# Scores of two attention heads as one block-diagonal product instead of two tile products

## The reference, cut to what matters

```python
B, H, S, D = 2, 8, 768, 64;  block, window = (32, 16)
k_sum = k.reshape(B, H, nb, block, D).max(axis=3)
v_sum = v.reshape(B, H, nb, block, D).mean(axis=3)
scores_l = np.where(np.abs(i - j) < window, scale * q @ k.T, -1e9)
scores_s = scale * q @ k_sum.T + np.log(block)
a = softmax(concatenate([scores_l, scores_s], axis=-1))
x = (a @ concatenate([v, v_sum])).transpose(0, 2, 1, 3).reshape(B * S, H * D)   # 1536 x 512
h = np.maximum(x @ w_in, 0.0);  x = h * h @ w_out                               # 512 -> 2048 -> 512
h = x @ w_in2;  out = P(h) / (Q(h) + 1e-6) @ w_out2                             # cubic over quadratic
```

## Time and profile before

| | us |
|---|---|
| median of three runs | 622.54 |
| lowest, highest | 621.97, 623.78 |
| the profiled execution's own time | 623.78 |
| its span, first to last instruction | 622.1 |
| TensorE busy in the span | 594.0 (95%) |
| VectorE, ScalarE, GpSimd busy | 443.7, 262.2, 144.5 |
| bytes moved by DMA | 35.54 MB, mean 57 GB/s |
| query loads | 8, 384.0 KB each, median 5.4 us from issue to landing |

### The profile page before, as it was taken

The page is one execution under the profiler, slowest core; times in us unless marked ns, Lnnn a source line. Parts: engine busy times, 40 slices in busy tenths (PEclk is TensorE's granted clock), DMA queues, the critical chain, the costliest instruction groups (busy, mean ns, idle before and its releaser), DMA issues.

```text
span 622.1 us, 9784 instructions
## 1 busy us (share of the span) xinstructions
PE 594.0 (95%) x3264; PEld 486.2 (78%) x3264; DVE 443.7 (71%) x862; ACT 262.2 (42%) x553; POOL 144.5 (23%) x144
## 2 busy tenths in 40 slices
PE   5878989999999999999999989999999999999995
PEld 4766768888888888888888867778888888888884
DVE  5656679667343333356666599999999999999996
ACT  4757731111131111130111755556756666765663
POOL 5435450000030000030000465622222222222220
PEclk9989999999999999999999999999999999999999
DMA  8999856000000000022222300000100000100001
GB/s 239 232 196 239 182 194 249 0 1 0 1 0 0 0 0 0 0 68 99 82 92 100 101 1 0 1 0 1 68 0 0 0 0 0 68 0 1 0 1 67
DMA packets 26973, 35.54 MB, mean 57 GB/s; under 512 B 1856, under 2 KB 19264, under 8 KB 26944
## 3 DMA queue, kind: packets, MB, share of 16 engines
q1 hardware_dynamic: 24544, 33.96, 19.4%
q10 hardware_dynamic: 2400, 1.18, 0.9%
HBM read 30.80 MB, written 3.15 MB: 55 GB/s over the span
## 4 chain that ended last, share of the span: by engine, by line
PE 47%; DVE 35%; issue 11%; POOL 3%; DMA 1%; ACT 1%; DVEq 1%; POOLq 0%
PE bank L479 22%; PE bank L536 21%; DVE ratio L941 9%; DVE numer L923 6%; DVE ratio L935 5%; DVE numer L921 5%; DVE ratio L930 5%; DVE hhi L948 4%; POOL kwin L318 2%; PE bank L434 2%; POOL prob L340 1%; DMA vwin<-vsum 1%; PE bank L444 1%; PE bank L452 1%; PE bank L465 1%
## 5 line engine op out<-in xcount | busy, mean ns | idle before, releaser
L479 PE MATMUL bank<-xhi,whi 128*128 (+1 forms) x384 | 149.7, 390 | 1.2 <-DVE wlo L829 1.2
L479 PE MATMUL bank<-xlo,whi 128*128 (+1 forms) x384 | 149.4, 389 | 0.0
L479 PE MATMUL bank<-xhi,wlo 128*128 (+1 forms) x384 | 149.4, 389 | 0.0
L632 ACT ACTIVATE hsq<-bank 128x512 f32<-128x512 f32 x48 | 28.7, 598 | 218.6 <-PE bank L479 218.6
L394 POOL TENSOR_TENSOR denom<-denom,habs 128x512 f32<-128x512 f32 (+1 forms) x49 | 62.3, 1272 | 250.9 <-ACT denom L703 250.9
L479 PEld LDWEIGHTS bank<-xhi,whi 128*128 128x128 f32 x384 | 72.1, 188 | 16.3 <-DVE wlo L829 1.4
L479 PEld LDWEIGHTS bank<-xlo,whi 128*128 128x128 f32 x384 | 72.1, 188 | 15.0
L479 PEld LDWEIGHTS bank<-xhi,wlo 128*128 128x128 f32 x384 | 72.1, 188 | 15.0
L551 PE MATMUL bank<-whi,hhi 128*128 128x512 f32 x192 | 75.9, 395 | 7.6 <-DVE hlo L952 7.6
L536 PE MATMUL bank<-hhi,whi 128*128 128x512 f32 x192 | 74.8, 390 | 0.1
L551 PE MATMUL bank<-wlo,hhi 128*128 128x512 f32 x192 | 74.9, 390 | 0.0
(11 more groups left out here) (67 smaller groups left out, 889.2 us busy)
## 6 DMA issues: line engine op xcount, KB each, us to landing
wraw<-w SPq DMA_DIRECT2D x32, 512.0 KB, 3.6
kraw<-kT SPq DMA_DIRECT2D x8, 384.0 KB, 7.9
q<-qT SPq DMA_DIRECT2D x8, 384.0 KB, 5.4
vnat<-v SPq DMA_DIRECT2D x8, 384.0 KB, 7.0
vwin<-v SPq DMA_DIRECT2D x8, 384.0 KB, 5.7
out<-osb SPq DMA_DIRECT2D x12, 256.0 KB, 2.1
vwin<-v SPq DMA_DIRECT2D x16, 88.0 KB, 5.9
vwin<-vsum ACTq DMA_DIRECT2D x8, 144.0 KB
```

What stands on the lines that cost most here:

```text
L479: last = mm(hps[j % 2][:, :], W[a][:, j, kt * P:(kt + 1) * P], X[b][:, kt, bass.ds(CH * c, CH)], start=k == 0, stop=k == 3 * KT - 1)
```

## The change

The scores of both heads of a window become one product. The stationary operand is a 128x128 matrix with head 0's 64 queries in the upper left block, head 1's in the lower right and zeros elsewhere; the moving operand is the whole of `kwin` for that window. The output rows are the same as before.

The query tile becomes `qblk`, of 128 x 128 x 12 numbers, with the window as the last index, so that the 12 windows of one query column lie side by side; the host lays the queries out in the same way. A load is two DMAs, one per diagonal block, into 64 partitions each, and TensorE waits for 32 instead of 16. The zero blocks are cleared once: for the first batch element on VectorE, ahead of the clearing of `vwin` (`cleared` then counts to 3), for the second on GpSimd, after the first windows. TensorE's first three rounds are now a loop in the program instead of three copies.

```diff
-        q.append(area(f"q{s}", [P, S]))
+        qblk.append(area(f"qblk{s}", [P, P, NW]))
...
+    def clear_queries(engine, s, h):
+        engine.memset(qblk[s][QW * h:QW * h + QW, QW * (1 - h):QW * (1 - h) + QW, :], 0.0).then_inc(cleared, 1)
...
         def load_q(it, s):
-            sp.dma_start(q[s][:, :], pick(qT, it, s)).then_inc(q_in[s], 16)
+            for h in range(2):
+                sp.dma_start(qblk[s][QW * h:QW * h + QW, QW * h:QW * h + QW, :],
+                             pick(qT, it, s)[QW * h:QW * h + QW]).then_inc(q_in[s], 16)
...
-        sp.wait_ge(cleared, 1)
+        sp.wait_ge(cleared, 3)
         load_vwin(0, 0, False)
...
         pool.wait_ge(windows_ready, 1)
+        for h in range(2):
+            clear_queries(g, 1, h)
+            pool.wait_ge(cleared, 4 + h)
         windows(0, 1, first=True)
...
             if gi == 0:
-                pe.wait_ge(q_in[s], 16 * (it + 1))
+                pe.wait_ge(q_in[s], 32 * (it + 1))
...
-                for h in range(2):
-                    rows = slice(D * h, D * h + D)
-                    last = mm(sps[par][QW * h:QW * h + QW, u * COLS:(u + 1) * COLS], q[s][rows, QW * w:QW * w + QW],
-                              kwin[s][rows, w, :], start=True, stop=True)
+                last = mm(sps[par][:, u * COLS:(u + 1) * COLS], qblk[s][:, :, w], kwin[s][:, w, :],
+                          start=True, stop=True)
...
         scores(0, 0, 2)
-        for it in range(PAIRS - 1):
+        pe.wait_ge(cleared, 5)
+        with pe.Fori(0, PAIRS - 1) as it:
             attention(it, False)
...
             d.memset(kraw[s][:, BAND + S:], 0.0)
+        for h in range(2):
+            clear_queries(d, 0, h)
...
+    def by_query(t):
+        return np.ascontiguousarray(features_first(t).reshape(PAIRS, B, P, NW, QW).swapaxes(3, 4))
...
-    arrays = {"qT": features_first(q), "kT": features_first(k), "v": tokens_first(v),
+    arrays = {"qT": by_query(q), "kT": features_first(k), "v": tokens_first(v),
```

More of the change, by code:

```diff
@@ L112, in build @@
     half = FT // 2 * SLOT * 4
-    q, kraw, kwin, vwin, vnat = [], [], [], [], []
+    qblk, kraw, kwin, vwin, vnat = [], [], [], [], []
     for s in range(B):
         area = Area((W_HI, W_LO)[s] + half)
-        q.append(area(f"q{s}", [P, S]))
+        qblk.append(area(f"qblk{s}", [P, P, NW]))
         kraw.append(area(f"kraw{s}", [P, S + 2 * BAND]))
@@ L323, in windows @@
             if first:
-                pool.wait_ge(cleared, 1)
+                pool.wait_ge(cleared, 3)
             else:
@@ L519, in _ @@
         pe.wait_ge(consts, 4)
-        pe.wait_ge(cleared, 1)
+        pe.wait_ge(cleared, 3)
         scores(0, 0, 0)
```

## The result

| | before | changed |
|---|---|---|
| median, us | 623.16 | 642.05 |
| lowest to highest, us | 621.97 to 631.94 | 640.87 to 645.67 |
| span of the profiled execution, us | 622.1 | 640.1 |
| first feed-forward matmul starts, us | 83.08 | 99.69 |

A forecast was written before the change was run, and what follows sets the result against it. The change was to act only on the attention, the first 86 us, bound by DMA stalls and a second loop. Matmuls -1.2 and query loads +2.0, all else zero, made +0.8: 623.3 us, range 620.5 to 628.5.

The forecast's parts named there:

- the strided load: Score weight loads, columns 48 bytes apart: taken as hidden behind matmul records, zero cost, at most +0.83 us a group.
- the rival: Score weight loads: strided load shows, 0.4 us a group, 6.6 us in all, 629.1 us; chance 0.13.
- The matmuls: Score groups on TensorE: eight full-size records in the old time, 0.12 us gained a group by tile shape, -1.2 us.
- the first part of the prediction: What bounds the kernel: the change acts on the attention, first 86 us, its gain or loss passed on one for one.
- The query loads: Attention's query DMAs, two to 64 partitions for one to 128: 0.4 us each, five count, +2.0 us (0 to +4.2).
- The two later stalls: Attention outputs waiting for the summary broadcast: ends expected at 38.2 and 58.2 us for 37.23 and 56.74.
- Rival (a): Query DMAs: narrow loads pay in full, +5.0 on six loads, less 1.2 makes +3.8, 626.3 us; chance 0.2.
- The clearing and the loop: VectorE and GpSimd clearing zero blocks, TensorE's rounds as loop: both 0; uncovered 1.4 us, and 0.3 if branches show.
- Rival (c): Attention: matmuls count, loads do not, and the low clock after the second stall goes: -3.0, 619.5 us; chance 0.12.
- Rival (d): Scores on TensorE: the gap before scores stays and the loads cost their 2.0: 624.5 us; chance 0.1.

The follow-up runs named there:

- e1: Changed kernel, score matmuls reading 128 adjacent columns instead of columns 48 bytes apart (scores wrong): 625.13 us, ratio 1.0038 to the kernel before.
- e9: Changed kernel with one query DMA to all 128 partitions and adjacent stationary columns (scores wrong): 622.29 us, ratio 1.0007 to the kernel before.
- e3: Kernel before with each query load split into two DMAs, to partitions 0 to 63 and 64 to 127: 625.90 us, ratio 1.0065.
- e10: Changed kernel with one query DMA to all 128 partitions, column distance 12 kept (scores wrong): 640.66 us in one execution.
- e4: Changed kernel with TensorE's first three rounds unrolled again: 641.87 us, ratio 1.0315 to the kernel before.
- e6: Changed kernel with queries in blocks of two windows, stationary columns 8 bytes apart, true scores: 627.69 us, ratio 1.0060 to the kernel before.
- e7: Changed kernel with queries in blocks of four windows, stationary columns 16 bytes apart, true scores: 637.99 us, ratio 1.0230 to the kernel before.

## Why the prediction was wrong

**The step that failed** is in the part on the strided load: "A load may last as long as a record, 0.10 us, before it shows", and "A load twice as slow is still hidden". The condition was right. The size was not: the load takes 0.263 us from start to start, five times the 0.05 that the prediction had worked out for adjacent columns (e1 shows only that these take 0.111 or less), so 0.15 us shows on each of eight records. In all that is +1.24 us from scores to outputs (2.22 against 0.98 in e1_adjacent), where I took zero.

**The bounds failed too.** I took +0.83 a group as the upper end, from a score group at the low clock, and halved it for the rival. A slow clock is another mechanism, and its price bounds nothing about a load's reads. No row of before held a strided load; the honest upper end was open, and the range should have leant that way. The rival's arithmetic was sound (three groups with a summary, TensorE alone): with the measured 3.32 a group, 3 x 3.32 + 1.42 = 11.4 us against 8.28, +3.1 eight times, makes 25 us, and I had put +0.8.

**From 27 to 16.6 us.** The first two score groups take 4.62 us where they took 3.46, the other 22 cost 1.16 each: 26.7 us. Given back are TensorE's waits of before, 9.3 us before 115 (5.8 for vwin<-vsum of the earlier trace rows, and by the same view of groups 0.4 for VectorE, 2.4 for POOL, 0.7 for ScalarE), of which 1.2 remain, and the 1.6 us of low clock in the earlier trace rows. 26.7 - 8.1 - 1.6 = 17.0; measured 16.6. A slower TensorE hid the DMA that had limited the attention.

**The matmuls** were right in kind: eight records in the old time, the idle time of 0.17 gone, 0.49 for 0.58 from transposes to scores. The gain was 0.08 us a group and not 0.12: only the way into scores, 0.09, came back, and eight records take 0.98 us to the outputs where sixteen took 0.97. What reaches the median cannot be told from nothing (e9). And the attention's gain is not "passed on one for one", as the first part of the prediction has it: in e9 half of it went to the low clock behind it.

**The query loads** were mis-sized, within their range: +2.0 forecast, +4.0 in kernel before (e3, 2.2 to 5.9), and 2 to 3 beside adjacent full-size matmuls (e1 against e9, not clear of noise). In the changed kernel itself they cost about nothing, since nothing waits for them there (e10). The two later stalls that I expected to end at 38.2 and 58.2 us do not exist in it; e3 has them at 37.72 and 59.46. Rival (a) priced the loads at +5.0 and, less the matmuls, the whole at +3.8; measured are +4.0 for the loads alone and +2.4 (0.6 to 4.2) for the whole without the strided loads (e1). Both lie between its price and the forecast's, and the runs cannot choose.

**The clearing and the loop** at zero were right as far as can be told (e9, e4). VectorE's two took 0.70 us each ahead of its key reduction, at 4.02 us (4.08 before), and GpSimd's, in the timeline of the changed kernel, 1.52 together, with 5.17 us of waiting for keys behind them:

```profile
6.35 1.52 POOL L221 MEMSET qblk<- 64x768 f32 x2
```

Rival (c) did not happen in the changed kernel: the earlier trace rows's slow group has no counterpart there, but because TensorE never rested. Its mechanism is seen in e9, where the stall before that group is 0.96 us instead of 2.85, the group runs at the full clock and the attention ends 2.9 us sooner, near its 3.0; what it left out is that the slow clock came back behind it. Rival (d) is refuted by the 0.49.

## What to carry to other kernels

Read the stationary operand with its columns adjacent, or at most 8 bytes apart for 32-bit data (0.05 us a group of eight loads here); a layout with an index inside the column's makes weight loads the bound of short matmuls. Where a cost is in no row, do not borrow another mechanism's price as its upper end: say that it is open, and ask what the kernel costs if the hidden thing is five times as long. In a DMA-limited stage, judge a layout by its bytes, its runs and its partitions first: each of the three cost more here than the matmuls could give.

## What the runs showed of the hardware that was not expected

- A 128-column load of 32-bit numbers takes 0.111 us or less from start to start at distance 1 (hidden behind the matmul), at most 0.118 at 2 (e6: eight within 1.02 us, one 0.196 long), 0.175 at 3, 0.23 at 4 ((1.94 - 0.33) / 7 in e7) and 0.263 at 12.
- A product of 128x128 with half of it zeros costs the same as two of 64x64 side by side, 0.98 and 0.97 us for four windows. There was nothing to gain in the arithmetic, only the change of shape, 0.09 us.
- Two DMAs of 64 partitions were slower than two of 128 with the same bytes and the same number of issues, by 3 us (ratios 1.0065 and 1.0015, whose intervals touch at 1.0035), and interleaving the partitions did not clearly mend it.
- A gain in one stage can be taken back by the clock of the next: in e9 the attention ended 2.9 us sooner, and the first 3.5 us of feed-forward matmuls ran at a granted clock of 0.53.
